# Attention stage on one core: rank products moved behind the scores into another PSUM bank, slot reads moved between the two mask products

## The reference

```python
for t in range(S):                      # q, k, v: (4, 8, 768, 64)
    state = gamma * state + einsum('bhd,bhe->bhde', k[:, :, t], v[:, :, t])
    y[:, :, t] = scale * einsum('bhd,bhde->bhe', q[:, :, t], state)
logits = x @ w_gate                     # x: (3072, 512), 8 experts
e_idx = np.argmax(logits, axis=1)
for e in range(E):
    mask = e_idx == e
    out[mask] = gate_w * eom * (relu(x[mask] @ w1[e]) @ w2[e])
return (silu(xn @ w_gate) * (xn @ w_val)) @ w_out
```

## Time and profile before

| what | us |
|---|---|
| median of 3 runs | 1107.06 |
| the three runs | 1105.83, 1107.13, 1107.06 |
| the profiled execution's own time | 1104.48 |
| its span | 1102.7 |
| TensorE busy in the span | 1088.8 (99%) |
| VectorE busy | 442.5 (40%) |
| ScalarE busy | 378.7 (34%) |
| GpSimd busy | 177.7 (16%) |

### The profile page before, as it was taken

One profiled execution on the slowest core, in us unless ns is written; L12 is line 12 of the kernel. 1 busy time (PEld: TensorE's weight loads), 2 busy tenths in 40 slices (PEclk: granted clock), 3 DMA queues, 4 the chain that ended last, 5 costly groups with the idle time before them and its releaser, 6 DMA issues.

```text
span 1102.7 us, 20452 instructions
## 1 busy us (share of the span) xinstructions
PE 1088.8 (99%) x6307; PEld 907.5 (82%) x6308; DVE 442.5 (40%) x886; ACT 378.7 (34%) x619; POOL 177.7 (16%) x245
## 2 busy tenths in 40 slices
PE   7999999999999999999999999999999999999998
PEld 6888887888888888887888888888888888888887
DVE  4777766342514425432433323423333243333222
ACT  3555534343525445433224231331133132213112
POOL 2444414222211211000010300210030011001000
PEclk9999999999999999999999999999999999999999
DMA  9999816333435434432101210111021001101001
GB/s 216 254 264 256 232 59 229 123 124 114 124 114 190 164 114 144 155 88 83 58 10 29 77 34 5 38 38 38 0 76 24 14 28 48 38 0 39 1 1 39
DMA packets 114069, 101.53 MB, mean 92 GB/s; under 512 B 81856, under 2 KB 87392, under 8 KB 114016
## 3 DMA queue, kind: packets, MB, share of 16 engines
q1 hardware_dynamic: 98752, 66.07, 22.1%
q0 software_dynamic: 8832, 26.81, 7.7%
q10 hardware_dynamic: 6432, 7.96, 2.1%
HBM read 76.41 MB, written 20.22 MB: 88 GB/s over the span
## 4 chain that ended last, share of the span: by engine, by line
PE 97%; issue 1%; DMA 1%; ACT 0%; POOL 0%; DVE 0%; SPq 0%; POOLq 0%
PE bank L730 15%; PE bank L731 15%; PE bank L732 15%; PE banks L654 14%; PE bank L627 14%; PE banks L730 3%; PE banks L731 3%; PE banks L732 3%; PE bank L538 2%; PE banks L524 2%; PE bank L568 2%; PE bank L576 1%; PE banks L642 1%; PE bank L618 1%; PE banks L517 1%
## 5 line engine op out<-in xcount | busy, mean ns | idle before, releaser
L1409 DVE TENSOR_TENSOR gated<-bank,sig 128x512 f32<-128x512 f32 (+1 forms) x78 | 50.7, 650 | 340.1 <-ACT sig L1022 337.1
L1022 ACT ACTIVATE sig<-bank 128x512 f32<-128x512 f32 x72 | 43.1, 598 | 325.4 <-PE bank L732 315.8
L730 PE MATMUL bank<-xh,w1h 128*128 128x512 f32 x384 | 149.4, 389 | 0.0
L731 PE MATMUL bank<-xl,w1h 128*128 128x512 f32 x384 | 149.4, 389 | 0.0
L732 PE MATMUL bank<-xh,w1l 128*128 128x512 f32 x384 | 149.4, 389 | 0.0
L1031 ACT ACTIVATE hh<-prod 128x512 fp32r<-128x512 f32 (+1 forms) x78 | 46.7, 599 | 109.9 <-DVE prod L1417 105.9
L730 PEld LDWEIGHTS bank<-xh,w1h 128*128 128x128 f32 x384 | 72.1, 188 | 15.0
L732 PEld LDWEIGHTS bank<-xh,w1l 128*128 128x128 f32 x384 | 72.1, 188 | 15.0
L731 PEld LDWEIGHTS bank<-xl,w1h 128*128 128x128 f32 x384 | 72.1, 188 | 14.9
L1176 DVE TENSOR_TENSOR hidl<-bank,hidh 128x512 fp32r<-128x512 f32 x29 | 20.1, 692 | 130.3 <-ACT hidh L881 130.3
L1423 DVE TENSOR_TENSOR hl<-prod,hh 128x512 fp32r<-128x512 f32 (+1 forms) x78 | 50.9, 652 | 51.2 <-ACT hh L1031 48.4
(11 more groups left out here) (243 smaller groups left out, 2139.5 us busy)
## 6 DMA issues: line engine op xcount, KB each, us to landing
stage<-in_moe_w SPq DMA_DIRECT2D x64, 512.0 KB
expert_rows<-tile_o ACTq DMA_DIRECT2D x29, 256.0 KB
q_raw<-in_q SPq DMA_DIRECT2D x24, 256.0 KB
k_raw<-in_k SPq DMA_DIRECT2D x24, 256.0 KB
v_raw<-in_v SPq DMA_DIRECT2D x24, 256.0 KB, 5.0
stage<-stage SPq DMA_DIRECT2D x64, 64.0 KB, 2.0
stage<-in_moe_w_out SPq DMA_DIRECT2D x6, 512.0 KB
stage<-in_moe_w_gate SPq DMA_DIRECT2D x5, 512.0 KB
```

The lines of the kernel that those rows point to most:

```text
L730: pe.matmul(out_ap, lh, rh, start=first, stop=False)
L731: pe.matmul(out_ap, lh, rl, start=False, stop=False)
L1022: nc.scalar.activation(sig[:], bank[GV[f % 2][0]][:, :], ACT.Sigmoid).then_inc(s["sig_done"], 1)
L1409: v3.tensor_tensor(gated[:, part], bank[GV[f % 2][0]][:, part], sig[:, part], ALU.mult)\
```

## The change

In steps 2 to 23 the rank products of unit u-2 go behind the scores of unit u. For units 0 to 21 they are written to columns 384 to 391 of the bank Y0, and so wait for the evacuation of the outputs of unit u-1 (`xT_out`); the products that write Y0 next wait for `slots_ready`. On VectorE, `place` goes between the two mask products. In `outputs`, the waits for the masked scores and for v go from before the state part to behind it. The wait of the gate logits for `slots_ready` is kept at two units only.

```diff
         def ranks_at(u):
             at = UNITS * 2 * EXPERTS
-            return bank[LOG][:, at:at + EXPERTS]
+            return bank[LOG if u > UNITS - 3 else Y0][:, at:at + EXPERTS]
...
             def outputs(u):
                 carried = u % CHUNKS > 0
-                pe.wait_ge(s["masked"], 2 * (u + 1))
-                pe.wait_ge(v_in[u % RAW], 16 * (u // RAW + 1))
                 if u:
                     pe.wait_ge(s["xT_out"], u)
+                if u > 1:
+                    pe.wait_ge(s["slots_ready"], u - 1)
                 if carried:
...
+                pe.wait_ge(s["masked"], 2 * (u + 1))
+                pe.wait_ge(v_in[u % RAW], 16 * (u // RAW + 1))
                 for a in range(2):
...
                 if u:
                     pe.wait_ge(s["onehot_ready"], u)
+                if u in (LEAD_UNITS + 1, UNITS - 1):
                     pe.wait_ge(s["slots_ready"], u)
...
                 state_sum(u)
+                scores(u)
                 if u == 2:
                     pe.wait_ge(s["mats_set"], 4)
                 if u > 1:
+                    pe.wait_ge(s["xT_out"], u)
                     ranks(u - 2)
-                scores(u)
...
-            def mask_scores(u):
+            def mask_scores(u, g):
                 if u > 1:
                     dve.wait_ge(s["y_done"], u - 1)
                 causal = ...
-                for g in range(2):
-                    dve.wait_ge(s["scores_done"], 2 * u + g + 1)
-                    v3.tensor_tensor(probs[:, u % 2, g:HEADS:2, :], quad(SC0 + g), causal, ALU.mult)\
-                      .then_inc(s["masked"], 1)
+                dve.wait_ge(s["scores_done"], 2 * u + g + 1)
+                v3.tensor_tensor(probs[:, u % 2, g:HEADS:2, :], quad(SC0 + g), causal, ALU.mult)\
+                  .then_inc(s["masked"], 1)
...
                 copy_state(u)
+                mask_scores(u, 0)
                 if u > 1:
                     place(u - 2)
-                mask_scores(u)
+                mask_scores(u, 1)
```

## The result

The changed kernel takes 1115.49 us (median of 4 runs, 1114.23 to 1117.29), the kernel before 1107.10 on the same chip (4 runs, 1105.83 to 1107.26). The ratio is 1.0080, 95% interval 1.0062 to 1.0097: slower by 7 to 11 us. 1112.2 was predicted, with a range of 1106 to 1117. 0.5 of the 11.5 is the start of the first q turn, 7.99 against 7.48; it lies between 7.4 and 8.8 over the 13 profiles of this case, whatever the kernel, so it is spread and no effect of the change.

The account below looks back on a forecast made before the run. PE's list of work was taken as the bound, with 97% of the span on PE. Terms -1.1 + 5.0 + 1.0 + 0.2 = +5.1 us on the median of 1107.06 gave 1112.2 us, range 1106 to 1117.

Parts of the forecast that it names:

- the forecast's: Main case in the attention: some 5 to 7 scatters late, 1109.3 to 1115 us, chance 0.61.
- every step held: Rival: nearly all scatters take 6 us, costing 0.5 us a step over 20 steps; 1116 us, chance 0.12.
- The scatter's delay: GpSimd's scatter, with slots ready between the masks, starts at 100.47 instead of 99.01, 1.46 us later.
- The known late scatters, 5 x 1.0, and 1.0 for the others: Row buffer: five seen late scatters hold the k turn 1.0 us each, 5.0 in all; all other scatters 1.0 us.
- The spare of 0.26 us: Between the end of the evacuation of turned x and the k turn waiting for it: 0.26 us at most.
- PE's order, -1.1: PE's weight loads: one tile shape change fewer around the rank products, 0.05 us a step, 22 steps, 1.1 us less.
- the best case: PE's order: the 0.13 us between the rank products and the scores goes in 22 steps, 2.9 us.
- The edits costed at nothing: Later second mask, moved waits on PE, and slots read before L517 asks for them: 0 us.
- The rank products' own wait, costed at 0: On PE, waiting for the evacuated outputs, an evacuation needed anyway for L576 right behind: 0 us.
- The end of the stage, 0.2: Gather of the first expert tile, queued on GpSimd behind a scatter, moves by 1.5 us; cost taken as 0.2 us.
- Landing unmoved: Rival: the scatter's transfer lands no later though issued later, so the holds vanish; 1107 us, chance 0.17.

Follow-up runs that it names:

- a_third_lead_waits: Changed kernel with a third row buffer, first expert's count also in bank Y0, waits for masked scores and v back ahead of L517: 1105.06 us, ratio 0.9979.
- a_lead: Changed kernel, two row buffers kept, first expert's count also written to bank Y0 so the gate logits skip the slots wait in step 22: 1114.96 us, ratio 1.0064.
- a_first: Changed kernel with the three slot operations ahead of both mask products instead of between them: 1109.91 us, ratio 1.0025 to the kernel before.
- b_late1: Kernel before, orders kept, scatter of unit u-2 held back until the first mask product of unit u is done: 1116.88 us, ratio 1.0074.
- b_late2: Kernel before, orders kept, scatter of unit u-2 held back until both masks of unit u are done: 1117.04 us, ratio 1.0100.

## Why the prediction was right, and where its sizes were off

The mechanism that decides was the one forecast: slots between the masks, scatter 1.5 us later, evacuation held by the transfer, k turn held by the evacuation. The number was nearer than the sum deserves. By its own bands 1115.49 lies not in the forecast's (1109.3 to 1115) but at the lower edge of the one for "every step held", which did not happen. On the profiled execution +5.1 us was forecast and +11.5 measured: of the difference 2.1 are holds that were longer, 1.4 a wait and 3.2 a clock that stood in no term, and 0.9 more than forecast came off through PE's order; the rest is small. So 4.6 of the 11.5 us came by paths that the sum did not have, and that the time lies inside the range owes something to luck and to the range's width. Point by point:

- *The scatter's delay.* 1.46 us worked out, 1.55 measured (1.53 against -0.02).
- *The known late scatters, 5 x 1.0, and 1.0 for the others.* This is the term that was mis-sized: 6.0 us forecast, 8.1 us measured, in nine holds. The number of holds was near (5 to 8 forecast), seven of the nine have the forecast size of 0.5 to 1. What was missed is the one of 3.2 us in step 4. The transfer of unit 0, which took 4.6 us before (22.37 to the completion at 26.92), took 8.2 after, started at 24.30. Taking the transfer's length as fixed failed in both directions: the lengths in the changed kernel run from 2.8 to 8.2 us, those of before from 3.7 to 6.5, with the same mean of 5.0 (units 0 to 19). So here a later issue did not shift each landing one for one; the transfers came out with another set of lengths.
- *The spare of 0.26 us.* The k turn follows the evacuation by 0.04 to 0.05 us, so 0.2 of it was true spare.
- *PE's order, -1.1.* In the trace -2.0, 0.09 us in each of 22 steps. The 0.13 us ahead of the scores does go, as the best case had it, and 0.03 to 0.04 comes back behind them. The Trainium skill (TensorEngine Tiling (Array Packing), Key Properties) says that a change of tiling mode drains TensorE. With one change fewer and the trace's 0.17 us for one, an estimate of 0.17 us a step would go; the step shows 0.09.
- *The edits costed at nothing.* Right for the masks, v, and the slots ahead of L517 (no wait of PE at L517 or L526 in steps 2 and on, and a_third_lead_waits). Wrong for a wait that was not worked out at all: the gate logits of unit 21 keep their wait for `slots_ready`. Of the three readers of the slots (scatter, L517, gate logits) only the first two were followed. It cost 1.4 us, because in that step five more operations stand ahead of the slots on VectorE, and they now come 1.4 us after PE asks; before, they came 0.15 us ahead. The rank products' own wait, costed at 0, held nothing in the changed kernel, and 0.6 us once in the kernels where the other holds were gone.
- *The end of the stage, 0.2.* Nothing: the first tile's gather starts at 143.78, its reader on PE at 149.86, and PE does not wait for it.
- *Half clock.* Not in the sum. The prediction counted a hold at its own length, but two stretches of 3.4 us at 1.2 GHz cost 3.2 us more in the profiled execution. Of the 5 profiles of kernels with held k turns (after, a_lead, a_first, b_late1, b_late2) each has one or two such stretches before 150 us, 8 in all; of the 8 profiles of kernels without, none has. That they belong together is shown by this count. Which hold sets off which stretch is not.
- *The rivals.* "Every step is held" would need all scatters at 6 us; half the evacuations still waited for PE. "Landing unmoved" had beside it the estimate of 2.6 us from the Trainium skill (DMA: Bandwidth & Descriptors, Anatomy of one DMA). The traces have that length only where the DMA engines have room: 2.7 to 2.8 us for the last scatters of the kernel before, from 136.84, 141.55 and 148.55 on, at a DMA share of 0.25 to 0.53, and for one of the changed kernel, from 130.09 on, at 0.26.

## What to carry to other kernels

Before work is moved ahead of a step that issues a transfer, follow the transfer to whoever needs its buffer back, and compare the delay with the spare there; a spare of some tenths in a stage whose DMA share is near 1 is none. One more buffer took the tie away in every kernel here that got it, and it is a cheap test of whether the tie is the cause. It does not make the delay free: put the same delay into the kernel that has the extra buffer, and compare those two. When a wait on a semaphore is kept "for a few units only", work those units out too, since they are the ones with extra work ahead of the signal.

## What the runs showed of the hardware

A transfer of 256 KB that GpSimd scatters in 2 KB rows took 2.7 to 2.9 us from its issue where the DMA share was 0.25 to 0.59. Where the share was 0.68 or more, which is all but one of the units 0 to 19, it took 3.6 to 8.2 us; the mean over these 20 units is 5.0 in both kernels. A scatter on GpSimd that waited for VectorE's mask product beside its slots started 0.5 us later than the mask's end and the old 0.29 us add up to (b_late1, b_late2). Holds of PE can cost more than their length: one or two stretches of 3.4 us at the granted clock of 0.50 stand in the attention of every profile with held turns, about 1.6 us each, and in none without. In PE's order, three changes of tile shape became two, and a step became 0.09 us shorter.
